# Reordering the two hand-overs of an attention, mixture-of-experts and feed-forward kernel on one core

## The reference

```python
# attention: 4 batches, 8 heads, 768 positions, head size 64; each row sees 4 sink keys and a window of 128
keep = is_sink | in_window
scores = np.where(keep, scale * np.matmul(q, k.transpose(0, 1, 3, 2)), -1e9)
a = np.exp(scores - np.max(scores, axis=-1, keepdims=True)); a = a / (a.sum(-1, keepdims=True) + 1e-09)
x = np.matmul(a, v)                                   # then heads side by side: (3072, 512)
# mixture of 8 experts, one expert per token, F = 1024
logits = x @ w_gate + modality_bias[modality_id]
e_idx = np.argmax(logits, axis=1)
gate_w = softmax(logits)[np.arange(N), e_idx]
out[mask] = gate_w[mask, None] * (np.maximum(x[mask] @ w1[e], 0.0) @ w2[e])      # for each e
# feed-forward, 512 -> 2048 -> 512
h = x @ w_in
g = h * (1.0 / (1.0 + np.exp(-1.702 * h)))
return (g @ w_out).astype(np.float32)
```

## Time and profile before

| | us |
|---|---|
| median of 3 runs | 1119.26 |
| lowest and highest | 1118.54, 1119.34 |
| the profiled execution, whole | 1117.76 |
| its span, first to last instruction | 1115.8 |
| PE busy in the span | 1100.6 (99%) |
| DVE, ACT, POOL busy | 424.8, 377.8, 326.1 |
| mean granted clock of PE | 0.998 |

### The profile page before, as it was taken

The page is one execution under the profiler, slowest core; times in us unless marked ns, Lnnn a source line. Parts: engine busy times, 40 slices in busy tenths (PEclk is TensorE's granted clock), DMA queues, the critical chain, the costliest instruction groups (busy, mean ns, idle before and its releaser), DMA issues.

```text
span 1115.8 us, 18740 instructions
## 1 busy us (share of the span) xinstructions
PE 1100.6 (99%) x5952; PEld 942.0 (84%) x5953; DVE 424.8 (38%) x1089; ACT 377.8 (34%) x781; POOL 326.1 (29%) x441
## 2 busy tenths in 40 slices
PE   9999999999999999999999999999999999999998
PEld 9999999987888888888878888888888888888887
DVE  5566666685122233212264223223223222322222
ACT  3666666643222233222344222222222222222222
POOL 8888888645641212212121001001001001000100
PEclk9999999999999999999999999999999999999999
DMA  9999999237111133211142001001001000000101
GB/s 222 217 258 236 239 229 229 72 124 264 38 47 47 47 108 127 75 47 38 38 147 89 20 1 56 19 0 47 27 1 47 19 9 28 9 0 1 38 1 38
DMA packets 57392, 92.04 MB, mean 82 GB/s; under 512 B 7936, under 2 KB 32768, under 8 KB 57344
## 3 DMA queue, kind: packets, MB, share of 16 engines
q1 hardware_dynamic: 51584, 72.56, 24.3%
q0 software_dynamic: 5760, 18.89, 4.8%
HBM read 72.02 MB, written 19.41 MB: 82 GB/s over the span
## 4 chain that ended last, share of the span: by engine, by line
PE 91%; DVE 4%; ACT 2%; issue 2%; DMA 1%; ACTq 0%; DVEq 0%; POOL 0%; SPq 0%; POOLq 0%
PE psum L981 8%; PE psum L982 8%; PE psum L983 8%; PE psum L972 8%; PE psum L974 8%; PE psum L973 8%; PE psum L789 5%; PE psum L938 4%; PE psum L940 4%; PE psum L913 4%; PE psum L915 4%; PE psum L914 4%; PE psum L939 4%; PE psum L764 2%; PE psum L925 2%
## 5 line engine op out<-in xcount | busy, mean ns | idle before, releaser
L1643 DVE TENSOR_TENSOR g<-psum,g 128x512 f32<-128x512 f32 x96 | 66.3, 691 | 295.0 <-ACT g L1176 295.0
L1176 ACT ACTIVATE g<-psum 128x512 f32<-128x512 f32 x96 | 57.4, 598 | 307.5 <-PE psum L974 304.0
L972 PE MATMUL psum<-x2T,win_hi 128*128 (+1 forms) x384 | 149.6, 390 | 2.3 <-DVE g L1643 2.3
L981 PE MATMUL psum<-w_hi,gT_hi 128*128 128x512 f32 x384 | 151.3, 394 | 0.0
L983 PE MATMUL psum<-w_hi,gT_lo 128*128 128x512 f32 x384 | 149.6, 390 | 0.0
L982 PE MATMUL psum<-w_lo,gT_hi 128*128 128x512 f32 x384 | 149.6, 389 | 0.0
L974 PE MATMUL psum<-x2T,win_lo 128*128 (+1 forms) x384 | 149.5, 389 | 0.0
L973 PE MATMUL psum<-x2T,win_hi 128*128 (+1 forms) x384 | 149.4, 389 | 0.0
L721 POOL DMA_INDIRECT out<-o_out,out_rows x20 | 21.5, 1075 | 412.6 <-ACT o_out L1189 408.1
L789 PE MATMUL psum<-v_sb,pT 128*128 128x73 f32 x704 | 105.9, 269 | 2.4 <-DVE pT L1397 1.2
L1385 DVE CUSTOM_DVE_ANT_0 s_msk<-psum,mask_sb 128x260 f32<-128x260 f32 (+1 forms) x192 | 75.0, 403 | 70.6 <-PE psum L753 38.2
(11 more groups left out here) (229 smaller groups left out, 1988.5 us busy)
## 6 DMA issues: line engine op xcount, KB each, us to landing
qk_raw<-qkT SPq DMA_DIRECT2D x64, 384.0 KB, 8.2
stage<-w SPq DMA_DIRECT2D x12, 1024.0 KB, 6.8
x<-y_rows SPq DMA_DIRECT2D x24, 256.5 KB, 2.7
vT_sb<-vT SPq DMA_DIRECT2D x16, 384.0 KB, 9.4
v_sb<-vP SPq DMA_DIRECT2D x16, 384.0 KB
x_rows<-x_sb SPq DMA_DIRECT2D x16, 384.0 KB, 5.7
win_raw<-w_in SPq DMA_DIRECT2D x16, 256.0 KB, 10.3
stage<-w_out SPq DMA_DIRECT2D x4, 1024.0 KB, 6.6
```

The lines of the kernel that those rows point to most:

```text
L972: pe.matmul(bank, wh, hi, start=(c == 0), stop=False)
L981: pe.matmul(psum[:, OB[t], :], gh, hi, start=(f == 0), stop=False)
L1643: dve.tensor_tensor(g32[:, f % 2, :], psum[:, FB[f % 2], :], g32[:, f % 2, :], ALU.mult)\
```

## The change

All of it lies in the two hand-overs. Into the mixture of experts: the three operations that find the first expert are moved on DVE from ahead of the positions to behind them; the tokens are marked in two halves of 12 tiles, each with its own comparison, and the token sort waits for the halves and for the last 6 tiles' `oh_slot` apart; `keep_going` has 17, 10 and 4 products in place of 18, 11 and 2; the gate sort is cut in two, 12 products ahead of `turn_xs(0)` and 12 behind it.

Into the feed-forward: ACT takes the sigmoid of chunks 0 and 1 ahead of `wout_highs(0)`, and rounds them between quarters 0 and 1; DVE multiplies them ahead of `wout_lows(0)` and subtracts after `gated(last + 1)`, ahead of `wout_lows(1)`; PE's wait for `y_moved` ahead of the loop is gone; SP fetches the rows of group 1 ahead of quarters 2 and 3 of w_out, and for that POOL takes the row numbers of group 0 ahead of the last scatter.

```diff
+                if q == 2:
+                    rows_of(1)
+                    for t in range(GT):
+                        load_x2(1, t)
...
-            for g in range(1, GROUPS):
+            for g in range(2, GROUPS):
...
-            for k in range(3):
-                scatter(total + (k - 3))
...
+            for k in range(3):
+                if k == 2:
+                    take_rows(0)
+                scatter(total + (k - 3))
...
-            take_rows(0)
...
-            keep_going(18)
+            keep_going(17)
...
-                if t in (0, PRE):
-                    pe.wait_ge(ohs_ready, 1 + t // PRE)
+                if t in (0, HALF_N, PRE):
+                    pe.wait_ge(ohs_ready, (0, HALF_N, PRE).index(t) + 1)
...
-            keep_going(11)
+            keep_going(10)
+
+            def sort_gates(tiles):
+                for t in tiles:
+                    mm = pe.matmul(psum[:, O_ps[1], 0:2 * SLOTS], oh_slot[:, t, :],
+                                   tile_gate[:, t].rearrange("p a s -> p (a s)"), start=(t == 0), stop=(t == NTILE - 1))
+                return mm
 
             pe.wait_ge(heads_done, B * H + AHEAD)
             pe.wait_ge(gates_marked, 1)
-            for t in range(NTILE):
-                mm = pe.matmul(psum[:, O_ps[1], 0:2 * SLOTS], oh_slot[:, t, :],
-                               tile_gate[:, t].rearrange("p a s -> p (a s)"), start=(t == 0), stop=(t == NTILE - 1))
-            mm.then_inc(gates_ready, 1)
-            keep_going(2)
+            sort_gates(range(HALF_N))
+            keep_going(4)
...
             turn_xs(0)
+            sort_gates(range(HALF_N, NTILE)).then_inc(gates_ready, 1)
             up(0, 0)
...
-            pe.wait_ge(y_moved, last + 2 + PRIMED)
-            pe.sem_inc(waited_pe, 1)
...
+            sigmoid(0, 0)
+            sigmoid(0, 1)
             wout_highs(0)
+            round_chunk(0, 0)
+            round_chunk(0, 1)
             wout_highs(1)
-
             act.wait_ge(y_ready, last + 2)
-            gate_chunk(0, 0)
-            gate_chunk(0, 1)
             wout_highs(2)
             wout_highs(3)
...
-            then(dve.scalar_tensor_tensor(out=e_cnt[:, 0, :], in0=count, scalar=0.0, in1=from_end[:],
-                                          op0=ALU.is_gt, op1=ALU.mult))
-            then(dve.tensor_reduce(e_cnt[:, 1, 0:1], e_cnt[:, 0, :], AX.X, ALU.max))
-            dve.tensor_scalar(first_e[:], e_cnt[:, 1, 0:1], -1.0, float(E), ALU.mult, ALU.add).then_inc(expert_known, 1)
...
+            then(dve.scalar_tensor_tensor(out=e_cnt[:, 0, :], in0=count, scalar=0.0, in1=from_end[:],
+                                          op0=ALU.is_gt, op1=ALU.mult))
+            then(dve.tensor_reduce(e_cnt[:, 1, 0:1], e_cnt[:, 0, :], AX.X, ALU.max))
+            dve.tensor_scalar(first_e[:], e_cnt[:, 1, 0:1], -1.0, float(E), ALU.mult, ALU.add).then_inc(expert_known, 1)
...
-            slot_row, slots = row(iota_row[:, 0:SLOTS], [P, NTILE, SLOTS]), [P, NTILE, SLOTS]
-            then(dve.tensor_tensor(tile_eq[:], slot_row, col(pos_t[:], slots), ALU.is_equal))
...
+                shape = [P, tiles.stop - tiles.start, SLOTS]
+                then(dve.tensor_tensor(tile_eq[:, tiles, :], row(iota_row[:, 0:SLOTS], shape),
+                                       col(pos_t[:, tiles], shape), ALU.is_equal))
+                dve.tensor_tensor(tile_tok[:, tiles, :], tile_eq[:, tiles, :], col(iota_tok[:, tiles], shape),
+                                  ALU.mult).then_inc(ohs_ready, 1)
+
+            mark_tokens(slice(0, HALF_N))
+            mark_tokens(slice(HALF_N, NTILE))
...
+            gate_product(0, 0)
+            gate_product(0, 1)
             wout_lows(0)
+            gated(last + 1)
+            chunk_low(0, 0)
+            chunk_low(0, 1)
             wout_lows(1)
-            gated(last + 1)
-            gate_chunk(0, 0)
-            gate_chunk(0, 1)
```

More of the change, by code:

```diff
@@ L95, in program @@
     assert QT * VW <= BANK and PRE * E <= RANK_AT and RANK_AT + (QT + 2) * E <= BANK and 0 < EARLY_AT < QT and 2 * E <= LW and VEXT <= VW and H % SLOT == 0
-    HALF_T = QT // 2
+    HALF_T, HALF_N = QT // 2, NTILE // 2
     PIECES = 4
@@ L1170, in x2_high, with sigmoid @@
                    .then_inc(x2T_high, 1)
-            def gate_chunk(g, f):
+            def sigmoid(g, f):
                 n = g * F2C + f
@@ L1177, in gate_chunk, with round_chunk @@
                    .then_inc(sig_ready, 1)
+            def round_chunk(g, f):
+                n = g * F2C + f
                 act.wait_ge(g_ready, n + (1 + G_FREE))
@@ L1180, in gate_chunk @@
                 act.copy(gT_hi[:, f % 4, :], g32[:, f % 2, :]).then_inc(gT_high, 1)
+            def gate_chunk(g, f):
+                sigmoid(g, f)
+                round_chunk(g, f)
             def move_out(g):
@@ L1481, in _ @@
             then(dve.tensor_tensor(pos_t[:], pos_t[:], rank_t[:, 0:NTILE], ALU.add))
-            slot_row, slots = row(iota_row[:, 0:SLOTS], [P, NTILE, SLOTS]), [P, NTILE, SLOTS]
-            then(dve.tensor_tensor(tile_eq[:], slot_row, col(pos_t[:], slots), ALU.is_equal))
-            def mark_tokens(tiles):
-                return dve.tensor_tensor(tile_tok[:, tiles, :], tile_eq[:, tiles, :],
-                                         col(iota_tok[:, tiles], [P, tiles.stop - tiles.start, SLOTS]), ALU.mult)
-            mark_tokens(pre).then_inc(ohs_ready, 1)
-            mark_tokens(own)
+            then(dve.scalar_tensor_tensor(out=e_cnt[:, 0, :], in0=count, scalar=0.0, in1=from_end[:],
+                                          op0=ALU.is_gt, op1=ALU.mult))
+            then(dve.tensor_reduce(e_cnt[:, 1, 0:1], e_cnt[:, 0, :], AX.X, ALU.max))
+            dve.tensor_scalar(first_e[:], e_cnt[:, 1, 0:1], -1.0, float(E), ALU.mult, ALU.add).then_inc(expert_known, 1)
+            slots = [P, NTILE, SLOTS]
+            def mark_tokens(tiles):
+                shape = [P, tiles.stop - tiles.start, SLOTS]
[5 more added lines that the diff above has]
+            mark_tokens(slice(HALF_N, NTILE))
             then(rows_in_tile(own))
@@ L1637, in x2_low, with gate_product @@
                                   hi[:, :, t * P:(t + 1) * P].bitcast(F32), ALU.subtract).then_inc(x2T_split, 1)
-            def gate_chunk(g, f):
+            def gate_product(g, f):
                 n = g * F2C + f
@@ L1644, in gate_chunk, with chunk_low @@
                    .then_inc(g_ready, 1)
+            def chunk_low(g, f):
+                n = g * F2C + f
                 dve.wait_ge(gT_high, n + 1)
@@ L1647, in gate_chunk @@
                                   ALU.subtract).then_inc(gT_split, 1)
+            def gate_chunk(g, f):
+                gate_product(g, f)
+                chunk_low(g, f)
             def move_out(g):
```

## The result

The changed kernel takes 1120.83 us in the median of 11 runs (1119.15 to 1123.69), the kernel before 1118.81 in 11 runs beside it (1117.27 to 1120.22). The ratio is 1.0023, with an interval of 1.0013 to 1.0032: slower by 2.0 us, where 1.4 us faster was forecast. Its profiled execution took 1119.15, the fastest of its 11 runs, with a span of 1117.2 against 1115.8: 1.4 us of the 2.0 can be read in the two traces.

The account below looks back on a forecast made before the run. PE, busy 99% of the span, was taken as the bound, so only its waits could be won. Terms -2.5 + 0.5 + 0.6 = -1.4 us took 1119.26 to 1117.9; the 8-in-10 range was 1116.3 to 1119.7.

Parts of the forecast that it names:

- The gain of -2.5: Feed-forward hand-over: PE's wait ahead of the third `ffn_up` vanishes, starting it at 583.54 in place of 586.04.
- The term of +0.5: Feed-forward: moved rows delay w_out's last quarter, so PE waits 0.5 us for chunk 2's multiplication, bounds 0 and 1.2.
- the DMA term: Feed-forward: the rows' delay of w_out, 2.2 to 2.5 us; too small if chunk 4's `ffn_up` waits over 1.5 us.
- The third rival: Feed-forward: POOL's row-number copies miss their gap, PE waits 3.3 us, sum +1.4, 1120.7 us; chance 10 in 100.
- The term of +0.6: Experts' hand-over: second `up`, held by w2's last quarter, moves from 263.53 by +0.6 us, between +0.2 and +1.1.
- Both DMA terms: Experts: first gather beside w1's tail +0.2 (0 to 0.5); second gather taking its share from w2 +0.2 (0 to 0.4).
- The second rival: Experts: PE's clock falls in the thin stretch ahead of the second `up`, +1.5 us, 1119.4; chance 12 in 100.
- the fall at 246: Experts: PE at 1.2 instead of 2.4 GHz for 246 to 249.5 before the change, priced at 1.5 us.
- the three DMA terms: Feed-forward w_out wait +0.5 (0 to 1.2); experts' first gather +0.2 (0 to 0.5) and w2 load +0.2 (0 to 0.4).

Follow-up runs that it names:

- a1: Kernel before with the change's whole hand-over to the feed-forward, hand-over to the experts as before; 1120.01 us, ratio 1.0005.
- a2: Kernel before with only the change's new order of chunks, group 1's rows and POOL's row numbers where they were before; 1116.95 us, ratio 0.9982.
- b1: Changed kernel with `relu(0)` and `xs_high(1)` ahead of the rounding of w2's last quarter on ACT; 1118.21 us, ratio to the kernel before 0.9992.
- b3: Changed kernel with seven idle products on PE behind `turn_xs(1)`, their result unread; 1121.44 us, ratio to the kernel before 1.0023.
- c1: Kernel before with only `first_e`'s three operations moved behind the positions; 1119.15 us, ratio 1.0004.
- a4: Kernel before with the change's experts' hand-over, but `first_e` ahead of the positions as before; 1121.15 us, ratio 1.0012.
- b2: Kernel before with the new chunk order and only group 1's first row tile and its row number moved early; 1115.93 us, ratio 0.9971.
- c2: Kernel before with only the gate sort cut in two around `turn_xs(0)` and its `keep_going` counts; 1121.36 us, ratio 1.0023.
- c3: Kernel before with only the tokens marked in two halves and the token sort waiting for them; 1119.39 us, ratio 1.0007.
- a3: Kernel before with the change's whole hand-over to the experts, feed-forward hand-over as before; 1121.58 us, ratio 1.0014.
- b4: Kernel before with new chunk order, one early row tile, and `relu(0)`, `xs_high(1)` ahead of w2's last quarter on ACT; 1115.95 us, ratio 0.9969.
- c4: Changed kernel with `relu(0)`, `xs_high(1)` ahead of w2's last quarter on ACT and only one early row tile; 1114.18 us, ratio 0.9967.

## Why the prediction was wrong, point by point

**The gain of -2.5 was right.** `down` gave way at 583.59 on the clock of before, against a forecast of 583.54, with both multiplications over in time.

**The term of +0.5 failed, and the step is the DMA.** Each step up to it held: POOL's first two copies ended at 578.0 and 580.2 as worked out, SP's first load went at 578.1 and the other three from 580.3. Then the prediction took the bytes of three loads at 320 to 364 GB/s, 2.2 to 2.8 us with the scatter, as the whole delay of w_out's last quarter. It was 3.9. Three loads of 0.34 with 0.13 between put quarter 2 at 581.78, 1.4 us later than before, and the last quarter then took 9.9 us to land instead of 7.4, another 2.5. How much of the 3.9 is SP's time to issue and how much the rate is not separated: the DMA was already moving 271 GB/s from 583 to 584 in the trace of after, as quarter 2 was being issued, and from 584 to 590 it moved 259 to 353 where before had 357 to 393. The last quarter was in at 592.3, not 590.3 to 590.9. From landing to PE it took 4.9, forecast 5.1, so 597.2, and PE wanted it at 595.1, forecast 594.9: 2.1 us of waiting, where 0.5 and at most 1.2 was forecast. The prediction named a wait of over 1.5 as the sign that the DMA term is too small, and a1 against a2 shows that the moved rows are the cause: with them 594.24, without them 588.75. The third rival gave 1120.7, close to the measured time, by luck: it had a wait of 3.3 us from copies that miss their gap, and the third and fourth copies ran as soon as the second was through.

**The term of +0.6 had the right mechanism and half the size.** `first_e` (241.05 on the clock of before, forecast 241.0), `gather_i` (246.08, forecast 246.1 to 246.2) and `turn_xs(0)` (251.59, forecast 251.5) came where they were put; the first `up` came at 254.48, forecast 253.9. The barrier moved by 1.2: 0.13 from the indices, 0.61 from the first gather (forecast 0.2, bound 0.5), 0.48 from w2's last load (forecast 0.2, bound 0.4). Both DMA terms lay beyond their upper bounds. The gather's is borne out by other runs: it took 4.15 to 4.3 us in the changed kernel, b1 and b3 and 3.84 in c1, which all load w1 late beside it, and 3.54 to 3.66 in before, a4, b2, c2 and c3. That w2's 0.48 is the second gather's doing is not shown, since the same load took 7.94 in b2, where that gather is issued nearly as late as before. The page DMA: Bandwidth & Descriptors of the Trainium skill, section on queues, rings and completion order, by which each engine takes turns between queues packet by packet, would have had the gather nearly on time; 4.15 against 3.54 us speaks against using it so.

**The clock was given 12 in 100, and that was the worst misjudgement.** The second rival described it: PE with only transposes until the barrier, then a full `up`, and the price 1.5. In the profiled execution it cost 0.7 (the third `turn_xs` is 1.90 later and the second `up` 1.23), in the runs probably more, since 9 of 11 of them have a clock of 0.996 or below and the profiled one has 0.997. The argument against it, that the 2.28 us of nothing at 586 cost no clock in the trace of before, rested on one execution. In other executions such a wait did cost it: a1 behind 2.57 us and b1 behind 2.38, each with products of 0.63, and in a4 and c2 the very wait of 2.28 us that was cited. One trace that shows no fall is not evidence that none falls. And the fall at 246, which the prediction takes as the fall of an idle PE, came after PE had been busy for 2.98 of the 3.00 us from 243 to 246; the wait of 1.07 us lay ahead of that.

**The sum.** In the traces the last `down` starts 1.60 later than before (1.84, less the 0.24 by which the stage starts earlier). With -2.45 and +2.07 at the feed-forward that makes +1.2, and the spans differ by 1.4; the 0.2 between is not placed. The rest, up to the 2.0 of the medians, is put down to the clock, which one trace of each kernel can't show. The losses of the two halves alone, a1 and a3, sum to 3.5 us by the medians and to 2.1 by the ratios; the change's 2.6 by ratio lies between.

**The range** of 1116.3 to 1119.7 missed because the bounds of the three DMA terms were too tight on the same side, and because the clock was a case of its own, where a gap of over 2 us in front of products of 512 columns should have made it part of every case.

**What stays open** is what decides, in one execution, whether the clock falls in such a gap. Filling the gap (b3) didn't show it, because the clock had fallen elsewhere and the third gather landed late.

## What to carry to other kernels

An operation that PE reaches earlier pays only if what ends the next wait moves too: read the chain of that wait, and move the barrier (here two lines on ACT, 0.31% by the ratios) before or together with the work in front of it. A load moved ahead of another can cost more than its bytes, here 3.9 us for three loads of 256 KB that were reckoned at 2.2 to 2.8; move only what the next consumer needs first, here one tile of four. A change that lengthens an idle gap in front of large products should be charged with a fall of the clock in a good part of its executions, and judged by many runs and not by one trace. Times of two traces should be counted from where their stage starts: here the starts lie up to 1.0 us apart, as much as several of the effects.

## What the runs showed of the hardware that was not expected

- A long wait of PE is followed in some executions by 2.6 to 3.4 us at half rate (products 0.43 apart instead of 0.23) and in others by none. Of the twelve waits of 2.0 us and more ahead of these products in the profiles, seven were followed by it: at the feed-forward those of a1, a4, b1, c2 (2.3 to 2.6 us) and b3 (3.88), at the experts those of a4 and the changed kernel. Not followed were those at the feed-forward of before, a3, c1, c3 (2.3) and the changed kernel (2.07). In c2 and c3 it also came behind 1.30 and 1.60 us. The runs of before with a mean clock of 0.996 or less lie 2.4 us above its others.
- In every profile the clock also fell over the sorts, where PE had work for most of the time, and there the fall is not free: the token sort took 2.82 to 2.88 us at full rate and 3.14 to 3.91 where the fall had reached it (a1, a2, a3, b3, b4, c2, c4).
- w2's last quarter took 7.52 us before and 7.96 to 8.18 in the kernels whose second gather is issued sooner behind it (c2, c3, a4, the changed kernel: 2.4, 2.0, 1.7 and 0.8 us, before 2.8), but also 7.94 in b2, at 2.7. So that the gather takes this time is suggested and not shown.
- The two quarters of w_out behind four loads of rows ran at 259 to 353 GB/s for 6 us and landed in 7.0 and 9.9 us (median 8.5; 9.1 in a1 and 8.3 in b1 with the same loads); behind one row tile (b2) the median landing is 6.6, as against 6.3 before. Why the rate is lower beside the rows was not isolated.
